# Low parts of the first gated block moved behind the next unit's first sum

## The reference

```python
k_p = k.reshape(B, H, Sp, pool, D).mean(axis=3)          # 576 keys -> 72, v likewise
attn = softmax(q @ k_p.T / sqrt(D)); x = attn @ v_p      # x: 2304 tokens x 512
xn = x / rms(x) * rms_g
x = (silu(xn @ w_gate) * (xn @ w_val)) @ w_out           # 512 -> 1536 -> 512, gated
h = x @ w_in                                             # 512 -> 2048
out = silu(h) @ w2_out                                   # 2048 -> 512
```

## Time and profile before

| what | value |
|---|---|
| median of 3 runs | 862.01 us (861.58 to 862.6) |
| the profiled execution, its own time | 862.45 us |
| its span, first to last instruction | 860.7 us |
| PE busy | 850.8 us, 99% |
| DVE / ACT / POOL busy | 551.4 / 360.0 / 421.2 us |
| mean granted TensorE clock | 0.999 |

### The profile page before, as it was taken

The page is one execution under the profiler, slowest core; times in us unless marked ns, Lnnn a source line. Parts: engine busy times, 40 slices in busy tenths (PEclk is TensorE's granted clock), DMA queues, the critical chain, the costliest instruction groups (busy, mean ns, idle before and its releaser), DMA issues.

```text
span 860.7 us, 13899 instructions
## 1 busy us (share of the span) xinstructions
PE 850.8 (99%) x5292; PEld 830.6 (96%) x5292; DVE 551.4 (64%) x835; ACT 360.0 (42%) x640; POOL 421.2 (49%) x415
## 2 busy tenths in 40 slices
PE   7999999999999999999999999999999999999998
PEld 6999999999999999999899899999999999999998
DVE  6689757875545579955664345569634798335873
ACT  3689845543221325545553221324333444134521
POOL 6898999883427480577763044380161700004300
PEclk9999999999999999999999999999999999999999
DMA  9971578778869987565779489997789748687762
GB/s 255 269 218 42 221 262 318 271 303 311 326 223 407 407 329 266 200 260 223 278 292 370 160 294 362 356 400 262 268 287 361 252 189 286 250 330 253 253 238 102
DMA packets 94801, 235.78 MB, mean 274 GB/s; under 512 B 23056, under 2 KB 69136, under 8 KB 83216
## 3 DMA queue, kind: packets, MB, share of 16 engines
q1 hardware_dynamic: 94736, 234.90, 75.9%
HBM read 164.10 MB, written 70.78 MB: 273 GB/s over the span
## 4 chain that ended last, share of the span: by engine, by line
PE 96%; DMA 2%; POOL 1%; DVE 0%; SPq 0%; issue 0%; DVEq 0%; POOLq 0%
PE ps L2001 17%; PE ps L2003 17%; PE ps L2002 17%; PE ps L2139 5%; PE ps L2138 5%; PE ps L2137 5%; PE ps L2099 3%; PE ps L2097 3%; PE ps L2098 3%; PE ps L1931 3%; PE ps L2068 3%; PE ps L2069 3%; PE ps L2067 3%; PE ps L2044 2%; PE ps L2043 2%; PE ps L2042 2%
## 5 line engine op out<-in xcount | busy, mean ns | idle before, releaser
L2001 PE MATMUL ps<-xh,wr 128*128 128x384 f32 x840 | 282.9, 337 | 0.3
L2003 PE MATMUL ps<-xh,wr 128*128 128x384 f32 x840 | 281.3, 335 | 0.0
L2002 PE MATMUL ps<-xl,wr 128*128 128x384 f32 x840 | 281.0, 335 | 0.0
L2001 PEld LDWEIGHTS ps<-xh,wr 128*128 128x128 f32 x840 | 157.6, 188 | 4.4 <-DVE qt L1570 1.5
L2002 PEld LDWEIGHTS ps<-xl,wr 128*128 128x128 f32 x840 | 157.8, 188 | 0.3
L2003 PEld LDWEIGHTS ps<-xh,wr 128*128 128x128 f32 x840 | 157.7, 188 | 0.0
L2138 PE MATMUL ps<-ew,efh 128*128 128x256 f32 x336 | 95.1, 283 | 0.0
L2139 PE MATMUL ps<-ew,efl 128*128 128x256 f32 x336 | 95.1, 283 | 0.0
L2137 PE MATMUL ps<-ew,efh 128*128 128x256 f32 x336 | 95.1, 283 | 0.0
L1589 DVE TENSOR_TENSOR qt<-ps,qt 128x384 f32<-128x384 f32 x84 | 46.4, 556 | 49.8 <-PE ps L2003 49.7
L950 POOL TENSOR_TENSOR eh<-eh 128x768 f32<-128x768 f32 x8 | 17.2, 2168 | 122.8 <-DVE efl L1666 122.8
(11 more groups left out here) (198 smaller groups left out, 1767.1 us busy)
## 6 DMA issues: line engine op xcount, KB each, us to landing
wr<-ring_home SPq DMA_DIRECT2D x40, 1792.0 KB, 9.7
ring_home<-wr SPq DMA_DIRECT2D x20, 1792.0 KB, 8.0
ew<-ending_home SPq DMA_DIRECT2D x8, 2048.0 KB, 8.5
out_home<-wo SPq DMA_DIRECT2D x14, 1024.0 KB, 9.4
fw<-fold_home SPq DMA_DIRECT2D x8, 1536.0 KB, 7.8
ew<-out_home SPq DMA_DIRECT2D x24, 512.0 KB, 7.2
fw<-out_home SPq DMA_DIRECT2D x18, 512.0 KB, 6.6
ending_home<-eb SPq DMA_DIRECT2D x16, 512.0 KB, 10.8
```

The lines of the kernel that those rows point to most:

```text
L2001: pe.matmul(out_ps, w_hi, x_hi, start=first and c == 0, stop=False, skip_group_check=True)
L2002: pe.matmul(out_ps, w_hi, x_lo, start=False, stop=False, skip_group_check=True)
L2003: ins = pe.matmul(out_ps, w_lo, x_hi, start=False, stop=c == 1, skip_group_check=True)
```

## The change

Two things move on VectorE, one on ScalarE. In the classic gated phase the low part of a group's first gated block (`low(n, 0)`) stood at the end of the V unit, ahead of the next unit's first sum; it now stands in the next unit behind `combine_u3`, ahead of the other three. In the fourth phase (`WHOLES[1]`, the third pair's first network) parts 0 and 2 of the first form's low parts stood at the end of the V units 7 and 9; they now stand in the G units 8 and 10, ahead of `combine_u3`. The high parts that they need, three copies on ScalarE, move from the end of G unit 6 into V unit 7, behind its `keep_first`.

```diff
@@ act_unit
+                if ph == WHOLES[1] and (letter, g) == ("V", PART):
+                    form_high(1, 0)
@@
-                if ph == WHOLES[1] and (letter, g) == ("G", PART):
-                    form_high(1, 0)
@@ dve_unit
+                if ph == WHOLES[1]:
+                    form_low(1, 0, {8: (0,), 10: (2,)}.get(x - first_unit[ph], ()))
                 combine_u3(x)
                 if x == 0:
                     scale_x(NT - 2)
                 if prior == 1 and classic[n - 1]:
+                    low(n - 1, 0)
                     low(n - 1, 1)
                     low(n - 1, 2)
                     low(n - 1, 3)
@@
                 if letter == "V":
                     gate(x, 2)
-                    if classic[n]:
-                        low(n, 0)
                 if ph in WHOLES:
                     e = WHOLES.index(ph)
-                    form_low(e, 0, ({9: (1,), 10: (2,)}, {7: (0,), 8: (1,), 9: (2,)})[e].get(x - first_unit[ph], ()))
+                    form_low(e, 0, ({9: (1,), 10: (2,)}, {8: (1,)})[e].get(x - first_unit[ph], ()))
```

## The result

| kernel | median | lowest to highest | profiled execution | its span |
|---|---|---|---|---|
| before, on the same chip | 862.14 us | 861.31 to 862.7 (12 runs) | 862.45 us | 860.7 us |
| changed | 864.41 us | 863.19 to 865.91 (12 runs) | 863.19 us | 861.4 us |

The changed kernel takes 1.0028 of the time before (95% interval 1.0021 to 1.0036), 2.3 us longer. That is more than the 0.2% (1.7 us) that the prediction called no change. The time lies inside its range.

The account below looks back on a forecast made before the run. TensorE, busy 850.8 of 860.7 us, was taken as the bound, so only its stalls counted. Gains of 1.12 us against costs of 2.10 made 0.98 longer, 863.0 us on the median of 862.01, range 861.2 to 864.5.

Parts of the forecast that it names:

- The bound: Whole kernel: TensorE busy 850.8 of 860.7 us, so time changes only where TensorE stands still for another length.
- edit 1: First phase, six units: the low part moved behind the sums gains at most 0.86 us in all.
- G4: First phase, gate unit of group 4: 0.36 us gained, called doubtful; cost 0.10 (0 to 0.3).
- G5: First phase, gate unit of group 5: 0.33 us gained, no cost.
- G1: First phase, gate unit of group 1: 0.07 us gained; down late by 1.55, between 1.05 (VectorE first) and 2.05 (POOL first).
- G2: First phase, gate unit of group 2: no stall to remove; cost 0.25 us at its down, ends 0 and 0.4.
- G3: First phase, gate unit of group 3: 0.10 us gained; cost 0.20 at its down.
- Edit 2: Fourth phase, form parts moved: 0.46 us gained at most, 0.25 cost, 0.20 net; ends 0.46 gained and 0.1 lost.
- Edit 3: Fourth phase, ScalarE's three form copies moved behind the copy of a product: 0.06 us gained, no cost.
- POOL goes first everywhere: Rival: first phase's low parts stand behind POOL, nothing gained in the fourth phase; 2.2 us longer, 864.2 us; chance 0.21.
- The cover holds: Rival: POOL and VectorE miss each other at the low parts, only gains stay; 1.4 us shorter, 860.6 us; chance 0.15.
- doesn't do what it says: Rival: G4's sum stays late, fourth phase exchanges stalls; 1.5 us longer, 863.5 us; counted within the forecast's chance of 0.60.

Follow-up runs that it names:

- e10: The changed kernel a second time, no edit of its own: 864.19 us, ratio 1.0028 to the kernel before.
- e3: Kernel before with the first phase's low part moved for groups 1 to 5 only, fourth phase as before: 861.78 us, ratio 0.9995.
- e6: Kernel before with only form part 0 and ScalarE's three copies moved, part 2 in its old place: 862.07 us, ratio 1.0000.
- e8: Kernel before with low parts moved for groups 3 and 4 only, form part 0 and copies moved, part 2 in old place: 861.47 us, ratio 0.9994.
- e4: Changed kernel plus POOL waiting ahead of line 883 in G1 until group 0's four low parts are done: 863.37 us, ratio 1.0015 to before.
- e1: Kernel before with all six low parts of the first phase moved as in the change, fourth phase as before: 863.41 us, ratio 1.0011.
- e5: Kernel before with the first phase's low part right behind the fourth gate, ahead of the second sum, in six units: 862.98 us, ratio 1.0010.
- e2: Kernel before with only the fourth phase's form parts and ScalarE's copies moved as in the change: 862.87 us, ratio 1.0008.
- e7: e2 plus POOL waiting ahead of its cast of the fifth ending weights until three form parts are done: 861.66 us, ratio 0.9996 to before.

## Why the prediction was wrong, point by point

**The bound.** Right. TensorE's busy time hardly changed (850.8 and 850.6 us), and the two phases that the change touches are longer by 2.06 of the 2.27 us (see the sum below).

**Gains of edit 1.** G4 and G5 were right to a few hundredths: 0.36 and 0.33 forecast, 0.32 and 0.30 found. In G4 the prediction chose rightly between two readings, but how the low part acts there is still open.

**Cost in G1: the first step that failed.** I had worked out both orders of the turns, 1.05 if VectorE stayed first and 2.05 if POOL went first, and I took 1.55, "the middle". (The terms given for the lower end, 0.43, 0.49 and two resumptions of 0.1, make 1.12 and not 1.05; the middle would be 1.58.) The middle is the cost of neither order, and all three executions profiled with edit 1 as it stands had POOL first. Nor was it quite open. The prediction said in the same place that the first low part led by 0.08 us and that POOL would come up to 0.3 earlier once the low part at 109.2 was out of its way. Counted from the start of the stretch, POOL's line 883 came 0.33 earlier (12.98 and 12.65 us behind 100.36 and 99.45), and the first low part only 0.03. "Up to 0.3" is more than 0.08, so POOL first was the likely end. The turn that the fourth gate now takes, 0.33 on line 873, stood in no term; it took back about half of what lines 869 and 870 gained. The prediction's working even gave the ends of the low parts: 114.7, 115.7, 117.3 and 118.9, less the 0.9 us by which the later execution was ahead, makes 114.8 for the second and 118.0 for the fourth, and the trace has 114.81 and 117.93, with the down beginning at 114.92 and going on at 117.99. Gain and cost together were to be 2.05 - 0.07 = 1.98 by this end; 1.85 was measured (1.88 in e10). The forecast had 1.55 - 0.07 = 1.48, so 0.37 too little.

**Costs in G2 to G4.** G2: 0.25 forecast, 0.21 found (0.10 in the stretch, 0.11 in the down). G3: 0.20 of cost less 0.10 of gain forecast; 0.02 gained was found (14.62 and 8.35 us against 14.67 and 8.32). In e10, the same code, it was 0.09. G4: 0.10 forecast, 0.02 found. These terms too hang on where POOL stands: in e3, with the same order on VectorE in these groups, G3 with its down takes 0.12 us more than before, and G4 with its down only 0.06 less. So G2 to G5 with their gains were to be 0.24 shorter and were 0.41 shorter.

**Edit 2: the second step that failed, and the larger one.** I forecast 0.20 gained, and the executions lost. Two things were wrong. The 0.46 to be gained was read from one execution. In the five others with part 2 in its old place the pause there is 0.11 at most, and the mean of the six is 0.10, so there was little to win. (Two of the five, e6 and e8, have the copies and part 0 moved.) And the cost was bounded by the cast, since I looked at the row of the cast alone. That bound itself was good (0.55; in e4, where the part does meet the cast, the pause was 0.51). But in the other three executions POOL came 0.7 to 1.2 us earlier than in the profile before, and there the next instruction in its queue, the 128x512 subtraction of line 939, was in the way. The four pauses have a mean of 0.93, so edit 2 costs about 0.8 us, and I had put 0.1 as its worst end.

**Edit 3.** 0.06 forecast. A pause of 0.11 us at 47.1 us of the phase (V unit 7) is in all four executions with the copies in their old place (before, e1, e3, e5) and in none of the eight with them moved. So the two moves that all eight share, the copies (edit 3) and part 0, gave 0.11. Part 0 starts only at 52.8 us in its old place, behind the pause, so it is the copies.

**The sum with the terms as measured.** First phase: 1.43 longer, where the forecast's terms make 1.48 - 0.24 = 1.24. Fourth phase: the four executions with form parts and copies as before (before, e1, e3, e5) have a mean of 80.94 us, and the four with both moved (changed, e2, e10, e4) one of 81.57, so 0.63 longer, where the forecast had 0.20 + 0.06 = 0.26 shorter. Together 2.06, against 0.98 forecast and 2.27 timed. Of the missing 1.1 us, 0.9 lie in the fourth phase and 0.4 in G1, and G2 to G5 give 0.2 back. The timing of e2 alone, 0.7 longer with an interval from 0.1 shorter to 1.5 longer, agrees with the 0.63 but can't show it; the stretches and e7 do.

**The rivals.** *POOL goes first everywhere* is what happened in G1; G2 lost 0.21, G3 and G4 next to nothing. Its 2.2 us and 864.2 us against 864.41 came out in part by luck: it had G2 to G5 with their gains at 0.26 longer where they were 0.41 shorter, and it had nothing gained in part 2 of the fourth phase, where 0.6 us were lost in all. The two errors, 0.7 each way, cancel. It got a chance of 0.21 because I held against it that G2 and G3 need misfortunes of their own. They were not needed: the decisive collision followed from the forecast's own numbers. *The cover holds* fell at once. Of *doesn't do what it says* the half about G4 fell by e8, and the half about the fourth phase came true: one stall was changed for another, and a larger one. The range, which took in the costly end, held.

**The signs that were named.** The new wait of the down on `DVE al L1611` was there in the first group, and gone in G4 and G5. The second group lost 0.21 us, but the view of waits names no wait on L1611 there, and the third lost nothing, where the sign wanted the first three. A stall before the sixth product in the fourth phase was there, larger than the one before the fourth that it replaced, which was named as a sign of being wrong. The first sum of G4 came 2.34 us behind the unit's start, as named. POOL's line 883 was not 1.6 us but 1.29 long: the mark of an instruction that went first.

The Trainium skill, "SBUF — State Buffer", section "SBUF: two separate sides", has the lock go to whoever starts first. The rows agree: line 883 took 1.29 us where it started first and 1.62 where the low part did, and the same four low parts took 5.61 us beside POOL and 1.95 without it. Applied to the 0.3 and the 0.08 us, it would have given the right case.

## What to carry to other kernels

When two engines take turns and the order hangs on less time than the edit itself moves, work out which way the shift goes and forecast that end. A value in the middle is the cost of neither order. Before an instruction is put into an idle gap of one engine, list everything that the other engine runs within a microsecond of it, not only the row that overlaps in one profile, because a start that hangs on a DMA moved by 1.9 us between executions here. And when a wait keeps the other engine away, see whether it has slack behind (the cast had, and the wait cost 0.1 us at most) or is full (as in G1, where the collision came back one group later).

## What the runs showed of the hardware that was not expected

- Four VectorE subtractions of 128x384 with both operands in SBUF took 1.95 us in a row with POOL waiting, 4.54 and 5.61 us with POOL at work. In these two stretches the engines alternate one for one: each subtraction ended 0.4 us behind one POOL instruction, whose row is 1.0 to 1.6 us long with its own wait in it.
- A VectorE subtraction of 128x768 took 0.95 us alone, 1.79 when it started 0.3 us into a POOL cast of 128x1024 (e4), and 2.05 when it started 0.3 us into a 128x512 subtraction. Both times it ended 0.8 us behind the POOL instruction.
- The same code ahead of it reaches the first phase between 98.94 and 101.44 us in different executions, a spread larger than the whole effect of this change. Two single profiles (0.74 us apart here) don't tell what twelve runs tell (2.27 us). Stretches from one matmul to another do repeat: 15.45 to 15.47 us in the three executions in which G1's low parts met POOL, and 14.67 to 14.72 in all the others but e5, where a part of the collision stands in the stretch (15.02).
